# Four ticks moved and the end of a data-dependent loop written once, in a fused attention, gated-layer and expert kernel on one Trainium2 core

## The reference

```python
# attention: q, k, v of [4, 8, 576, 64]; heads 0-3 local (the 32 keys up to the query),
# heads 4-7 strided (keys at multiples of 32 behind the query)
scores = where(masks, q @ k.T / 8, -1e9); attn = softmax(scores) @ v
x = attn.transpose(0, 2, 1, 3).reshape(2304, 512)
# gated layer
xn = x / sqrt(mean(x * x) + 1e-6) * rms_g
y = (silu(xn @ w_gate) * (xn @ w_val)) @ w_out        # 512 -> 1536 -> 512
# eight experts, one per token
logits = y @ router_w + modality_bias[modality_id]
e = argmax(logits); gate = softmax(logits)[e]
out = gate * (relu(y @ w1[e]) @ w2[e])                # 512 -> 1024 -> 512
```

## Time and profile before

| | |
|---|---|
| median of 3 runs | 880.37 us (880.21 to 880.69) |
| the profiled execution, its own time | 880.37 us |
| its span, first to last instruction | 878.6 us |
| mean granted clock of PE | 0.991 |
| attention head start, before the gated layer's first product | to about 54 us |
| gated layer with attention | to about 599 us |
| experts | to the end |

### The profile page before, as it was taken

The page is one execution under the profiler, slowest core; times in us unless marked ns, Lnnn a source line. Parts: engine busy times, 40 slices in busy tenths (PEclk is TensorE's granted clock), DMA queues, the critical chain, the costliest instruction groups (busy, mean ns, idle before and its releaser), DMA issues.

```text
span 878.6 us, 15595 instructions
## 1 busy us (share of the span) xinstructions
PE 859.4 (98%) x5233; PEld 738.0 (84%) x5242; DVE 520.6 (59%) x1400; ACT 374.3 (43%) x944; POOL 330.7 (38%) x372
## 2 busy tenths in 40 slices
PE   8989999999999999999999999999999999999995
PEld 5668898888888888899999999998888888888884
DVE  6974565333453335449787763883777447666662
ACT  6965413545454455543221132232456235555440
POOL 3835772345333443346346333070043112122221
PEclk9999999999999999999999999999999999999998
DMA  8983212222114210242121121626275646555520
GB/s 193 282 204 83 62 45 65 72 77 74 54 45 114 63 38 25 72 156 73 42 91 60 60 73 37 227 61 252 96 235 184 227 143 217 208 193 199 196 82 26
DMA packets 77517, 103.40 MB, mean 118 GB/s; under 512 B 38973, under 2 KB 43069, under 8 KB 77312
## 3 DMA queue, kind: packets, MB, share of 16 engines
q1 hardware_dynamic: 73760, 91.16, 33.5%
q0 software_dynamic: 3680, 11.28, 3.7%
HBM read 92.98 MB, written 10.22 MB: 117 GB/s over the span
## 4 chain that ended last, share of the span: by engine, by line
PE 89%; DVE 6%; POOL 2%; issue 1%; ACT 1%; DVEq 0%; POOLq 0%
PE ps L1232 32%; PE ps L1271 15%; PE ps L1790 13%; PE ps L1775 13%; PE ps L1163 3%; PE ps L1192 2%; PE ps L1173 2%; PE ps L1800 2%; PE ps L1139 2%; PE ps L649 1%; PE ps L1308 1%; DVE w_lo L2022 1%; PE ps L1301 1%; DVE w_lo L852 1%; DVE sm L1506 0%
## 5 line engine op out<-in xcount | busy, mean ns | idle before, releaser
L1024 POOL TENSOR_TENSOR sm<-sm,rinv 72x288 f32<-72x288 f32 (+1 forms) x51 | 45.6, 894 | 177.6 <-DVE rinv L1517 177.5
L1056 POOL TENSOR_TENSOR out_lo<-out_raw,out_hi 128x512 fp32r<-128x512 f32 x72 | 102.9, 1428 | 5.8
L1575 DVE SCALAR_TENSOR_TENSOR h<-h,ps 128x384 f32<-128x384 f32 x72 | 39.8, 553 | 105.5 <-ACT h L1423 104.4
L1054 POOL CAST out_hi<-out_raw 128x512 fp32r<-128x512 f32 x72 | 51.2, 712 | 133.9 <-DMA out_raw<-in_moe_w_out 133.9
L1232 PE MATMUL ps<-x_hi,val_hi 128*128 128x384 f32 x288 | 101.2, 351 | 0.0
L1232 PE MATMUL ps<-x_hi,gate_hi 128*128 128x384 f32 x288 | 100.6, 349 | 0.4 <-DVE h L1575 0.4
L1427 ACT ACTIVATE h_hi<-h 128x384 fp32r<-128x384 f32 x72 | 37.8, 525 | 141.3 <-DVE h L1581 141.3
L1232 PE MATMUL ps<-x_hi,gate_lo 128*128 128x384 f32 x288 | 97.3, 338 | 0.0
L1232 PE MATMUL ps<-x_hi,val_lo 128*128 128x384 f32 x288 | 96.5, 335 | 0.0
L1232 PE MATMUL ps<-x_lo,val_hi 128*128 128x384 f32 x288 | 96.4, 335 | 0.0
L1232 PE MATMUL ps<-x_lo,gate_hi 128*128 128x384 f32 x288 | 94.2, 337 | 0.0
(11 more groups left out here) (278 smaller groups left out, 1949.7 us busy)
## 6 DMA issues: line engine op xcount, KB each, us to landing
w_raw<-in_moe_w SPq DMA_DIRECT2D x72, 512.0 KB, 4.8
out_raw<-in_moe_w_out SPq DMA_DIRECT2D x72, 256.0 KB, 2.6
x_rows<-y_tiles SPq DMA_DIRECT2D x18, 256.0 KB, 2.6
early_w_raw<-in_moe_w SPq DMA_DIRECT2D x8, 512.0 KB, 7.1
gate_raw<-in_moe_w_gate SPq DMA_DIRECT2D x4, 768.0 KB, 8.3
val_raw<-in_moe_w_val SPq DMA_DIRECT2D x4, 768.0 KB, 10.5
qk<-in_q SPq DMA_DIRECT2D x8, 288.0 KB
qk<-in_k SPq DMA_DIRECT2D x8, 288.0 KB
```

What stands on the lines that cost most here:

```text
L1024: pool.tensor_tensor(s3, s3, rinv[0:n, i, :].unsqueeze(2).to_broadcast([n, 4, c]), ALU.mult).then_inc(s_no, 1)
L1054: pool.tensor_copy(oh[i][:, :], o_raw[i][:, :]).then_inc(s_oh, 1)
L1056: pool.tensor_tensor(ol[i][:, :], o_raw[i][:, :], oh[i][:, :].bitcast(f32), ALU.subtract).then_inc(s_ol, 1)
L1575: dve.scalar_tensor_tensor(out=hf[n % 2][:, :], in0=hf[n % 2][:, :], scalar=1.0, in1=ps[:, 0, 0:CH], op0=ALU.add, op1=ALU.mult).then_inc(s ...
```

## The change

Five edits, independent of each other:

- `ROUTER` goes from (3, 3, 1) to (3, 4, 0), so SP issues the router's load four ticks later, behind the rows read again for tile 0 and behind one more out block.
- `PLACE_1`, `IDX_1` and `GATHER_1` go forward by two ticks, two ticks and two ticks: the placing matmuls from in front of down to in front of val of f=7, the indices on DVE from (8, 0, 1) to (7, 2, 1), the gathers from (8, 1, 1) to (8, 0, 1).
- The nest only holds steps: `while_live` tests `n_used > t - 1` at each level and goes in. Behind it stands one `last`, for every engine, with the number `s` of the final slot from a register. `final` (a new table entry, `used` - 1) is made by DVE and loaded by each engine.
- POOL's `last` has a nest of its own, `arrived`, for the waits on gathers and scatters that only exist in live steps.
- DVE's evacuation of q and k at tick `QK_BY_ACT` - 1 goes from the head of the tick to where the other ticks have it.

```diff
--- before.py
+++ after.py
@@ -140,7 +140,7 @@
 
 
 DOTTED = TT * (NC - 3)
-ROUTER = at(NC - 3, 3, 1)
+ROUTER = at(NC - 3, 4, 0)
 PAUSE = (SPAN - 6, 0)
 DOT_TICKS = [s for s in range(at(NC - 3, 5, 0), at(NC - 1, 1, 0, 1)) if PAUSE[1] < (s - EARLY) % SPAN < PAUSE[0]]
 DOT = {(i, e): DOT_TICKS[(E * i + e) * len(DOT_TICKS) // (E * DOTTED)] for i in range(DOTTED) for e in range(E)}
@@ -175,7 +175,7 @@
 HOT_1, EXP_1, COUNT_1, GATE_1 = at(LC, 3, 2, 1), at(LC, 4, 0), at(LC, 4, 1), at(LC, 4, 1, 1)
 STAR_1, W_LOAD_1 = at(LC, 4, 2, 1), at(LC, 5, 0)
 SKIP_1, RANK_1, MARK_1, POS_1 = at(LC, 5, 1, 1), at(LC, 5, 2, 1), at(LC, 6, 1, 1), at(LC, 6, 2, 1)
-PLACE_1, IDX_1, GATHER_1 = at(LC, 7, 2), at(LC, 8, 0, 1), at(LC, 8, 1, 1)
+PLACE_1, IDX_1, GATHER_1 = at(LC, 7, 1), at(LC, 7, 2, 1), at(LC, 8, 0, 1)
 ROWS_1, ROWS_HI_1, ROWS_LO_1 = at(LC, 10, 0), at(LC, 10, 0, 1), at(LC, 10, 1, 1)
 W_SPLIT_AT = by_tick([((0, i), at(LC, 7 + i // 2, 2 * (i % 2), 0)) for i in range(4)]
                      + [((1, i), at(LC, 9 + i // 2, 2 * (i % 2), 0)) for i in range(4)])
@@ -299,6 +299,7 @@
         fresh = rx.put("fresh", [P, SLOTS], i32)
         nth = rx.put("nth", [P, SLOTS], i32)
         used = rx.put("used", [P, 1], i32)
+        final = rx.put("final_slot", [P, 1], i32)
         star_i = rx.put("early_expert", [P, 2], i32)
 
         rh = Region(gl_at, gl_at + QB)
@@ -588,17 +589,13 @@
         last_row = []
         route_steps = [0]
 
-        def to_the_end(eng, n_used, step, last, t):
-
-
-            if t == STEPS:
-                last(t - 2)
-            else:
-                with eng.If(n_used < t):
-                    last(t - 2)
-                with eng.Else():
-                    step(t, t % 4)
-                    to_the_end(eng, n_used, step, last, t + 1)
+        def while_live(eng, n_used, do, t=None):
+
+            t = SURE if t is None else t
+            if t < STEPS:
+                with eng.If(n_used > t - 1):
+                    do(t)
+                    while_live(eng, n_used, do, t + 1)
 
         def run(eng, step, last):
 
@@ -610,7 +607,9 @@
             for t in range(5 + 4 * whole, SURE):
                 step(t, t % 4)
             n_used = eng.value_load(used[0:1, 0:1], min_val=NTT, max_val=SLOTS)
-            to_the_end(eng, n_used, step, last, SURE)
+            s = eng.value_load(final[0:1, 0:1], min_val=NTT - 1, max_val=SLOTS - 1)
+            while_live(eng, n_used, lambda t: step(t, t % 4))
+            last(s, n_used)
 
         def live(t, lag):
 
@@ -1616,10 +1615,6 @@
 
             for s in range(TICKS):
                 c, f, sub, half = step_of(s) if s >= EARLY else (0, 0, -1, 0)
-                if s == QK_BY_ACT - 1:
-                    for key in QK_AT.get(s, []):
-                        dst, src = evac_qk(dve, *key)
-                        dve.tensor_copy(dst, src).then_inc(s_qe, 1)
                 if (sub, half) == (1, 0):
                     scale_gate(FT * c + f)
                 if (sub, half) == (2, 0):
@@ -1634,7 +1629,7 @@
                         dve.tensor_copy(dst, src).then_inc(s_qe, 1)
                 for j in SCORE_AT.get(s, []):
                     mask_max(j)
-                if EARLY <= s < QK_BY_ACT - 1:
+                if EARLY <= s < QK_BY_ACT:
                     for key in QK_AT.get(s, []):
                         dst, src = evac_qk(dve, *key)
                         dve.tensor_copy(dst, src).then_inc(s_qe, 1)
@@ -1742,14 +1737,20 @@
             for t in range(2, 5):
                 step(t, t % 4)
 
-            def last(s):
+            def arrived(t):
+                if live(t, -AHEAD):
+                    pool.wait_ge(s_xg[(t + AHEAD) % 4], 16 * ((t + AHEAD) // 4 + 1))
+                pool.wait_ge(s_out[t % 2], 16 * ((t - 2) // 2 + 1))
+
+            def last(s, n_used):
 
                 pool.tensor_copy(idx_last[:, :], idx_scatter[:, bass.ds(s, 1)]).then_inc(s_ilast, 1)
                 pool.wait_ge(s_ilast, 1)
                 for n in range(4):
-                    pool.wait_ge(s_xg[n], 16 * len(range(n, min(s + 2 + AHEAD, SLOTS), 4)))
+                    pool.wait_ge(s_xg[n], 16 * len(range(n, SURE + AHEAD, 4)))
                 for n in range(2):
-                    pool.wait_ge(s_out[n], 16 * len(range(n, s, 2)))
+                    pool.wait_ge(s_out[n], 16 * len(range(n, SURE - 2, 2)))
+                while_live(pool, n_used, arrived)
                 pool.wait_ge(s_yo, s + 1)
                 pool.nop(nofuse=True)
                 pool.indirect_dma_start(out=out[:, :],
@@ -2104,6 +2105,7 @@
             link(dve, dve.tensor_tensor(placed[:, 0, :], placed[:, 0, :], placed[:, 3, :], ALU.add))
             dve.tensor_copy(idx_scatter[:, EARLY_SLOTS:SLOTS], placed[:, 0, :]).then_inc(s_route, 1)
             link(dve, dve.tensor_scalar(used[:, :], incl[:, E - 1:E], float(EARLY_SLOTS), None, ALU.add))
+            link(dve, dve.tensor_scalar(final[:, :], incl[:, E - 1:E], float(EARLY_SLOTS - 1), None, ALU.add))
             link(dve, dve.tensor_scalar(live_f[:, :], slot_no[:, :], incl[:, E - 1:E], None, ALU.is_lt))
             link(dve, dve.memset(fresh_f[:, 0:1], 1.0))
             link(dve, dve.tensor_tensor(fresh_f[:, 1:SB], exp_f[:, 1:SB], exp_f[:, 0:SB - 1], ALU.not_equal))
```

## The result

The changed kernel is slower: 887.9 us as the median of 6 runs (885.62 to 891.18) against 880.39 (877.95 to 882.26) for the kernel before in the same comparison; ratio 1.0097 [1.0079, 1.0114]. The forecast was 882.7, at most 884.6: right in sign, a third of the size. Most of what is missing lies in one place, the last tile.

What follows compares the result with a forecast made beforehand. PE, busy 859.4 of 878.6 us, was taken to bound the kernel. From 880.37 us, 1.94 + 1.6 - 0.6 + 0.1 + 0.3 - 1.0 = +2.3 gave 882.7 us, range 880.2 to 884.6.

Steps and rivals of the forecast that it cites:

- Step 7: Exit of the nest: PE's far jump ahead of `last` costs +0.3 us (0 to 1); DVE's 2.8 us jump is hidden.
- rival B: PE's `last` lies across two instruction blocks, the second arriving late: 884.5 to 886.4 us; chance 0.07.
- Step 4: Router's weights: load issued later, landing at 390.5 at the earliest, cover shrinking from 2.6 to 0.3 us: +0.1 us.
- Step 1: Early placing matmuls ahead of val of f=7: PE waits for DVE's `at_pos`, +1.94 us.
- Step 2: PE's clock behind the placement wait: falls to 0.50 for a stretch, +1.6 us; 0 if it stays up.
- Step 3: Early indices on DVE: PE's stall for `scale_gate` at 577 goes, -0.6 us (0 to -0.7).
- Steps 5 and 6: Moved evacuation at `QK_BY_ACT`, and routing's added `final_slot` with one more register load per engine: 0 each.
- Step 8: The end: instruction fetch of DVE's exit jump falls sooner, so the last scatter lands sooner, -1.0 us.
- Rival D: GpSimd's final drain of 3838 ns is a wait for code and shrinks: 877.5 us (879.1 if the clock falls); chance 0.06.
- rival C: The placement wait does not appear, `at_pos` being ready: 879.8 us; chance 0.07.

Runs made afterwards that it cites:

- nest_dve_short: As nest_alone, but DVE's nest cut to four levels (19 to 22), the other engines keeping theirs: 880.35 us, ratio 0.9998.
- dve_copies: Nest and exit changed as in the changed kernel for PE, ACT and GpSimd; DVE keeps the old nest with a `last` at each level: 880.6 us, ratio 1.0.
- nest_pe_short: As nest_alone, but PE's nest alone cut to four levels: 884.75 us, ratio 1.0048.
- nest_alone: Changed kernel with the router and placement ticks of before, so single `last`, `final_slot` and the moved evacuation remain: 885.2 us, ratio 1.0048.
- place_three: Kernel before with only `PLACE_1`, `IDX_1` and `GATHER_1` moved: 883.18 us, ratio 1.0025.
- place_matmuls: Kernel before with only `PLACE_1` moved, ahead of the val matmuls of f=7: 884.91 us, ratio 1.005.
- index_alone: Kernel before with only `IDX_1` and `GATHER_1` moved: 879.95 us, ratio 0.9997.
- before_hold: Kernel before with one more wait at the end of DVE's `last`, for the last scatter's landing ahead of its far jump: 881.15 us, ratio 0.9992.

## Why the prediction was wrong

**Step 7, the nest and its exit, is the step that failed.** It had PE's jump right: it names 3.69 us and a loss of 0.3 from it, and the jump took 3.77 and ended at 865.8, some 0.4 us after PE ran dry. It had DVE's jump right too, 2.8 us, behind the `yo`. What it got wrong is "hidden, by 0.9". It asked only when DVE delivers hT_lo. But the first thing that DVE's `last` does is `split(s)`, and when the expert is not a new one that is nothing but the count on `s_w2l`; PE's `last` waits for that count ahead of its very first matmul (`pe.wait_ge(s_w2l, ...)`). Before, DVE gave it at 862.4, 0.5 us ahead of PE's first matmul of `last` at 862.95, so the cover of this count was 0.5 us. Now it stands behind the jump (864.6 to 867.4), a register load and two tests, at 868.6. Of 2.8 us of jump and 0.25 more of register load (0.56 us in place of 0.31) that cover leaves 2.5; the term was +0.3 and measured +2.6 in the profiles. PE's jump runs beside DVE's and adds nothing. nest_dve_short and dve_copies against nest_pe_short show it. The sentence of the Trainium skill that step 7 named ("Runtime: NRT & Kernel Launch", Instruction fetch mechanics) agrees with the far jumps of all fourteen profiles, 3.3 to 3.8 us on PE and 2.8 to 3.0 on DVE, and with 0.36 and 0.5 where the jump was cut short; rival B (a second block) did not occur.

**The clock behind that hole was not in the sum.** It follows from the first error: with a gap of 0.3 there was no reason for it, with 3.3 it came in all three profiles that have the hole (the changed kernel, nest_alone, nest_pe_short) and in none of the eleven others. It cost 1.5 us in the first and the last of them and 2.7 in nest_alone; by the means of nest_alone the clock part is 1.8.

**Step 4, the router, was mis-sized:** +0.1 stood for +1.4 in the profile and 1.1 ± 0.4 by the means. The chain (three copies, tanh, `scale_gate`, gate) was right to the tenth, and its 0.3 of cover too. The input failed: a landing of 7.1 us taken from another place in the queue. Fifteen of the sixteen parts did land after 7.3 us, the last after 8.7. The text had a landing up to 1 us later costing 0.7; it was 1.6 later. With all parts at 7.3 us the cover of 0.3 would just have held, so the loss is that of one late part.

**Step 1 held:** forecast 1.94, measured 1.95, 1.8 and 1.7. **Step 2** held in two of three profiles with this wait (place_three, place_matmuls), and not in that of the changed kernel; by the means of place_three the clock part is 1.0 of the 1.6. The choice between 0 and 1.6 is not one that a trace decides; it is a chance per execution.

**Step 3** held where the indices missed GpSimd's split (place_three, index_alone) and failed in the profile of the whole, where they met it: `scale_gate` was ready at 581.3 with PE there at 580.9. The step counted DVE's work as "the same in amount"; its durations depend on GpSimd. It also took the stall at 577 for one of order alone, while 2.5 us of DVE's time ahead of it were the same meeting.

**Steps 5 and 6** cost nothing that can be seen: dve_copies has both, and its rest is -0.4 ± 0.3. **Step 8** held in the profile: 3.8 us fell to 2.7, -1.2 at the end; before_hold, which has this gain alone, shows none by its means. Rival D did not occur, GpSimd's drain is 3838 ns in the changed kernel as before.

So of the 5.2 us that are not clock, the steps had 0.7; against their parts alone the nest lacks 3.4, the router 1.0 and the placement 0.3. The range was also drawn too narrow by its own working: rival C, at 879.8, lay below its lower end of 880.2, and most of rival B above its upper one.

## What to carry to other kernels

Before a far jump is moved ahead of the last work, list every semaphore that any engine's last work waits for and ask on which side of the signaller's jump it is given; a signal without data (a bare count) is the one that is overlooked. Where one engine has slack behind it and another waits at its side, the copies can be kept on the one and dropped on the others, which cost nothing here. And a wait of PE of some 3 us is to be priced with the half-clock stretch behind it: filling it with useless matmuls won 3.0 us by the medians, 2.5 by the means. Last, a second engine's operation of a few elements that takes 1.2 us in place of 0.17 in a profile is waiting: look at what GpSimd runs beside it before its place in the order is blamed.

## What the runs showed that was not expected

- The last scatter's landing goes by DVE's exit jump in all fourteen profiles: 3.2 to 3.9 us in the seven where DVE jumps while it is under way, 2.7 in the seven where the jump comes earlier or waits. In the former one of the sixteen parts comes late (in dve_copies fifteen by 873.80, the last at 875.04).
- The same figure appears in mid-kernel: beside a fetched block of instructions near 388 us a transfer's sixteenth part landed 1.2 to 1.5 us behind the others in eight of the fourteen profiles, and in six not. What decides it stays open.
- The profiled execution of nest_dve_short had no stretch at 0.50 between 7.6 and 867.8 us and a span of 873.8 us, 4.8 below its own median span. The kernel before ranged over 874.9 to 881.4 us at mean clocks of 0.996 to 0.986 in one group of 29. That spread of 6.5 us is larger than the mean cost of any single part here.
